# Two batches of retention one after the other, the first group's operands made within the second batch, and a new order of conversions, norm and banks

## The reference, cut to what matters

```python
# retention: q, k, v are (2 batches, 8 heads, 768 tokens, 64)
for t in range(S):
    state = gamma * state + einsum('bhd,bhe->bhde', k[:, :, t], v[:, :, t])
    y[:, :, t] = scale * einsum('bhd,bhde->bhe', q[:, :, t], state)
x = y.transpose(0, 2, 1, 3).reshape(1536, 512)
# first feed-forward layer, 512 -> 2048 -> 512
h = x @ w_in
x = (h * sigmoid(1.702 * h)) @ w_out
# norm and second, gated layer, 512 -> 1536 -> 512
xn = x / sqrt(mean(x * x) + 1e-6) * rms_g
g = xn @ w_gate
out = (g * sigmoid(g) * (xn @ w_val)) @ w_out2
```

## Time and profile before

| | us |
|---|---|
| median of three executions | 650.26 (646.29 to 654.38) |
| the profiled execution | 644.55 |
| its span | 642.8 |
| TensorE (PE) busy | 596.5, 93% |
| TensorE's weight loads (PEld) busy | 562.3, 87% |
| VectorE (DVE) busy | 348.4, 54% |
| ScalarE (ACT) busy | 309.9, 48% |
| GpSimd (POOL) busy | 172.4, 27% |

### The profile page before, as it was taken

The page is one execution under the profiler, slowest core; times in us unless marked ns, Lnnn a source line. Parts: engine busy times, 40 slices in busy tenths (PEclk is TensorE's granted clock), DMA queues, the critical chain, the costliest instruction groups (busy, mean ns, idle before and its releaser), DMA issues.

```text
span 642.8 us, 9071 instructions
## 1 busy us (share of the span) xinstructions
PE 596.5 (93%) x3486; PEld 562.3 (87%) x3486; DVE 348.4 (54%) x477; ACT 309.9 (48%) x533; POOL 172.4 (27%) x187
## 2 busy tenths in 40 slices
PE   8996899899998887899998897799999999999997
PEld 7885899899998886799998896798888999998886
DVE  4557455447634544547644555666575466566331
ACT  2444566654425663544435553457343555555331
POOL 2643255100122443000122343352012355440000
PEclk9998799999999998999999898999999999999999
DMA  8881122322221121221312121223221522223102
GB/s 321 273 318 60 34 67 65 99 67 66 65 63 37 33 67 40 67 91 38 93 34 56 44 66 33 66 67 91 75 66 34 165 65 68 85 80 81 50 0 99
DMA packets 24219, 52.83 MB, mean 82 GB/s; under 512 B 1776, under 2 KB 1904, under 8 KB 24176
## 3 DMA queue, kind: packets, MB, share of 16 engines
q1 hardware_dynamic: 24176, 52.25, 26.5%
HBM read 49.09 MB, written 3.15 MB: 81 GB/s over the span
## 4 chain that ended last, share of the span: by engine, by line
PE 80%; DVE 7%; issue 4%; ACT 4%; POOL 3%; DMA 1%; SPq 1%; ACTq 0%; DVEq 0%; POOLq 0%
PE bank L432 36%; PE bank L383 13%; PE bank L386 12%; PE bank L385 12%; ACT w_hi L501 2%; PE bank L329 2%; PE bank L357 2%; DVE w_lo L657 2%; PE bank L338 2%; DVE x L745 1%; POOL raw L898 1%; PE bank L351 1%; DMA arena<-attn_in 1%; POOL raw L896 1%; PE bank L479 1%
## 5 line engine op out<-in xcount | busy, mean ns | idle before, releaser
L657 DVE TENSOR_TENSOR w_lo<-raw,w_hi 128x512 fp32r<-128x512 f32 (+2 forms) x148 | 141.1, 955 | 145.4 <-ACT w_hi L501 144.7
L383 PE MATMUL bank<-x_hi,w_hi 128*128 128x384 f32 x560 | 193.9, 346 | 27.0 <-DVE bank L707 18.5
L385 PE MATMUL bank<-x_lo,w_hi 128*128 128x384 f32 x560 | 189.5, 338 | 0.0
L386 PE MATMUL bank<-x_hi,w_lo 128*128 128x384 f32 x560 | 189.4, 338 | 0.0
L501 ACT ACTIVATE w_hi<-raw 128x512 fp32r<-128x512 f32 (+2 forms) x148 | 112.9, 766 | 59.0 <-POOL raw L898 35.0
L383 PEld LDWEIGHTS bank<-x_hi,w_hi 128*128 128x128 f32 x560 | 106.9, 191 | 35.0 <-DVE bank L707 25.0
L385 PEld LDWEIGHTS bank<-x_lo,w_hi 128*128 128x128 f32 x560 | 107.1, 191 | 0.7 <-issue 0.6
L386 PEld LDWEIGHTS bank<-x_hi,w_lo 128*128 128x128 f32 x560 | 106.9, 191 | 0.0
L530 ACT ACTIVATE g_hi<-arena 128x768 fp32r<-128x768 f32 x56 | 46.8, 844 | 105.5 <-PE bank L432 105.5
L692 DVE TENSOR_TENSOR g_lo<-arena,g_hi 128x768 fp32r<-128x768 f32 x56 | 53.2, 956 | 79.3 <-ACT g_hi L530 79.1
L896 POOL TENSOR_TENSOR raw<-raw 128x256 f32<-128x256 f32 x40 | 30.0, 750 | 240.4 <-DVE w_lo L657 240.4
(11 more groups left out here) (64 smaller groups left out, 613.7 us busy)
## 6 DMA issues: line engine op xcount, KB each, us to landing
raw<-w SPq DMA_DIRECT2D x68, 512.0 KB, 3.7
arena<-attn_in SPq DMA_DIRECT2D x24, 512.0 KB, 6.2
out<-x SPq DMA_DIRECT2D x1, 1536.0 KB, 6.4
out<-x SPq DMA_DIRECT2D x6, 256.0 KB, 2.0
arena<-tables SPq DMA_DIRECT2D x1, 518.0 KB, 5.4
arena<-tables SPq DMA_DIRECT2D x1, 256.0 KB, 7.4
ident<-ident_in SPq DMA_DIRECT2D x1, 64.0 KB, 9.9
gain<-gain_in SPq DMA_DIRECT2D x1, 2.0 KB, 10.4
```

What stands on the lines that cost most here:

```text
L383: pe.matmul(dst, w_hi[q][:, w], x_hi[:, x], start=start and kk == 0, stop=False, skip_group_check=True)
L385: pe.matmul(dst, w_hi[q][:, w], x_lo[:, x], start=False, stop=False, skip_group_check=True)
L386: mm = pe.matmul(dst, w_lo[q][:, w], x_hi[:, x], start=False, stop=kk == 1, skip_group_check=True)
L657: dve.tensor_tensor(w_lo[q % 3][:, dst], src, w_hi[q % 3][:, dst].bitcast(F32), ALU.subtract)\
```

## The change

1. Retention goes batch by batch: step a is chunk a % 6 of batch a // 6. State, k and q decays are counted anew; the increment k^T v is made for each head by itself, 8 matmuls of 64 x 64 in place of 4 of 128 x 128. Each batch's first chunk has no cross part, each batch's last no increment.
2. The seven operands of group 0 are made between the steps of the second batch, and the weights of unit 0 are split and lowered behind them.
3. Hidden units: on VectorE `c22` comes ahead of the lowering of the unit's weight pieces 1 and 2, which moves into the unit that uses them; TensorE waits for piece 2 only ahead of product 7. GpSimd makes its four sums without waiting for a lowering, two of them into columns of their own, and the raw buffers are two of 1792 columns.
4. The norm's steps stand two units later and are spread out; the diagonals are two VectorE instructions of 768 columns with a high and a low part, and the broadcast uses four fp32r matmuls. The second half of `normalise` moves into the first project unit.
5. The hidden tiles 0 and 1 are converted earlier in a pass's last hidden unit. `FIRST` takes banks 0, 1, 6, 2 ahead of product 4.

```diff
...
-FIRST = {1: (6, 7, 0, 1, 2, 4, 3, 5), 2: (6, 7, 0, 1, 2, 4)}
+FIRST = {1: (0, 1, 6, 2, 4, 3, 5, 7), 2: (0, 1, 6, 2, 4, 7)}
...
                     for p in range(PAIRS):
-                        mm = pe.matmul(val[par][:, cols(p, P)], k_dec[par][:, cols(p, P)], v[:, cols(p, P)],
-                                       start=True, stop=True)
+                        for h in range(2):
+                            mm = pe.matmul(val[m % 2][64 * h:64 * h + 64, cols(p, 64)],
+                                           k_dec[m % 2][:, cols(2 * p + h, 64)], v[:, cols(2 * p + h, 64)],
+                                           start=True, stop=True, skip_group_check=True)
...
-                pe.wait_ge(w_lo_done, lo_at[r] + 3)
+                pe.wait_ge(w_lo_done, lo_at[r] + 2)
                 pe.wait_ge(m1_copied, n + 1)
                 product(6, n, 2, 1, 2, T2, False)
                 product(2, n, 0, 0, 2, B21, False)
                 pe.wait_ge(m5_copied, n + 1)
                 product(3, n, 1, 1, 3, B22, False)
                 pe.wait_ge(u2_copied, n + 1)
+                pe.wait_ge(w_lo_done, lo_at[r] + 3)
                 product(7, n, 2, 1, 0, T3, False)
...
-                    mm = pe.matmul(bank[6 + th][:, 0:HALF], ones[:, :], diag[:, cols(th, HALF)], start=True, stop=True)
+                    pe.matmul(bank[6 + th][:, 0:HALF], ones_r[:, :], diag_hi[:, cols(th, HALF)],
+                              start=True, stop=False)
+                    mm = pe.matmul(bank[6 + th][:, 0:HALF], ones_r[:, :], diag_lo[:, cols(th, HALF)],
+                                   start=False, stop=True)
                 mm.then_inc(bcast_done, 1)
-                    if p in (1, 2) and j == 2:
+                    if p in (1, 2) and j == 4:
                         norm_totals(p - 1)
-                    if p in (1, 2) and j == 4:
+                    if p in (1, 2) and j == 6:
                         norm_bcast(p - 1)
...
+                for c in {3: (B11,), 4: (B21,), 7: (T1,), 8: (T2, B22), 9: (T3,), 10: (T4,)}.get(a, ()):
+                    split_x(0, c)
+                if a == 10:
                     split_w(0, 0)
-                    split_w(0, 1)
-                if s == 10:
-                    split_w(0, 2)
-            for c in (T1, T2, B22, T3, T4):
-                split_x(0, c)
+            split_w(0, 1)
+            split_w(0, 2)
...
+                    if last:
+                        split_g(p, 0)
...
+                    if last:
+                        split_g(p, 1)
...
-                    if p in (1, 2) and j < 2:
-                        squares(p - 1, j)
-                    if j == HIDDEN[layer] - 1:
-                        split_g(p, 0)
-                        split_g(p, 1)
+                    if p in (1, 2) and j < 4:
+                        squares(p - 1, j // 2, j % 2)
...
-                for t in range(SEQ // P):
-                    ins = dve.tensor_scalar(diag[:, cols(t, P)], ident[:, :], inv_rms[:, t:t + 1], None, ALU.mult)
...
+                for diag, inv in ((diag_hi, inv_hi[:, :].bitcast(F32)), (diag_lo, inv_lo[:, :])):
+                    ins = dve.tensor_tensor(diag[:, :].rearrange("p (t q) -> p t q", q=P),
+                                            ident[:, :].unsqueeze(1).to_broadcast(shape),
+                                            inv.unsqueeze(2).to_broadcast(shape), ALU.mult)
                 ins.then_inc(diag_done, 1)
...
+                if c > 0:
+                    dve.wait_ge(state_decayed, (CHUNKS - 2) * g + c)
...
+                if a == 4:
                     lower_x(0, B11)
+                elif a == 5:
                     lower_x(0, B21)
-                if s == 10:
+                elif a == 6:
+                    sum_x(0, T1)
+                elif a == 7:
+                    sum_x(0, T2)
+                    lower_x(0, T1)
+                elif a == 8:
+                    lower_x(0, T2)
+                    lower_x(0, B22)
+                elif a == 9:
+                    lower_x(0, T3)
+                    sum_x(0, T4)
+                elif a == 10:
+                    lower_x(0, T4)
                     lower_w(0, 0)
-                    lower_w(0, 1)
-            lower_w(0, 2)
-            sum_x(0, T1)
-            lower_x(0, T1)
-            sum_x(0, T2)
-            lower_x(0, T2)
-            lower_x(0, B22)
-            lower_x(0, T3)
-            sum_x(0, T4)
-            lower_x(0, T4)
 
...
                         c22(n - 1)
-                        if is_val(n - 1):
-                            gate_tile(n - 1, 2)
-                            gate_tile(n - 1, 3)
-                    lower_next(r, 0)
+                    lower_w(r, 1)
+                    if j > 0 and is_val(n - 1):
+                        gate_tile(n - 1, 2)
+                    lower_w(r, 2)
+                    if j > 0 and is_val(n - 1):
+                        gate_tile(n - 1, 3)
+                    if p in (1, 2):
+                        if j in (2, 4):
+                            add_squares(p - 1, j // 2 - 1)
+                        if j == 5:
+                            means(p - 1)
+                        if j == 6:
+                            diagonals(p - 1)
+                        if j == 7:
+                            normalise(p - 1, 0)
+                    if j == HIDDEN[layer] - 1:
+                        lower_g(p, 0)
+                    lower_next(r)
                     if is_val(n):
                         gate_tile(n, 0)
-                    lower_next(r, 1)
                     c12(n)
                     if is_val(n):
                         gate_tile(n, 1)
-                    lower_next(r, 2)
-                    if p in (1, 2):
-                        if j < 2:
-                            add_squares(p - 1, j)
-                        if j == 3:
-                            means(p - 1)
-                        if j == 4:
-                            diagonals(p - 1)
-                        if j in (5, 6):
-                            normalise(p - 1, j - 5)
                     if j == HIDDEN[layer] - 1:
-                        lower_g(p, 0)
                         lower_g(p, 1)
...
-                    lower_next(r, 0)
-                    for f in (2 * j + 2, 2 * j + 3):
-                        if f < TILES[layer]:
-                            lower_g(p, f)
-                        if f == 2 and is_val(n):
-                            gate_tile(n, 3)
+                        if p in (1, 2):
+                            normalise(p - 1, 1)
+                    lower_next(r)
+                    if j < PROJECT[layer] - 1:
+                        lower_g(p, 2 * j + 2)
...
                 pool.tensor_tensor(s1, a21, a22, ALU.add).then_inc(w_sums, 1)
                 pool.wait_ge(w_sums, sums_at[r] + 1)
+                pool.tensor_tensor(s2, s1, a11, ALU.subtract).then_inc(w_sums, 1)
+                pool.wait_ge(w_sums, sums_at[r] + 2)
+                pool.tensor_tensor(s4, a12, s2, ALU.subtract).then_inc(w_sums, 1)
+
                 pool.tensor_tensor(a21, a11, a21, ALU.subtract).then_inc(w_sums, 1)
-
-                pool.wait_ge(w_lo_done, lo_at[r] + 1)
-                pool.wait_ge(w_sums, sums_at[r] + 2)
-                pool.tensor_tensor(a11, s1, a11, ALU.subtract).then_inc(w_sums, 1)
-                pool.wait_ge(w_sums, sums_at[r] + 3)
-                pool.tensor_tensor(a12, a12, a11, ALU.subtract).then_inc(w_sums, 1)
```

More of the change, by code:

```diff
@@ L68, in transformer_kernel @@
         w_lo = [sb(f"w_lo{i}", 1024, F32R) for i in range(3)]
-        raw = [sb(f"raw{i}", 1280) for i in range(3)]
+        raw = [sb(f"raw{i}", 1792) for i in range(2)]
         t3 = sb("t3", OPERAND)
@@ L294, in _ @@
             sp.dma_start(gain[:, :], gain_in).then_inc(const_in, 16)
-            for s in range(SLOTS, STEPS):
-                sp.wait_ge(y_done, s - SLOTS + 1)
-                load(s)
-                load_kv(s)
-                if s >= STEPS - 3:
-                    load_weights(s - STEPS + 3)
-            for r in range(3, len(units)):
+            for a in range(SLOTS, STEPS):
+                sp.wait_ge(y_done, a - SLOTS + 1)
+                load(a)
+                load_kv(a)
+                if a in (7, 9):
+                    load_weights((a - 7) // 2)
+            for r in range(2, len(units)):
                 load_weights(r)
@@ L571, in squares @@
                     act.wait_ge(sum_sq_done, 2 * i + th)
-                for dh in range(2):
-                    act.activation(square[dh][:, :], x32[i][:, cols(2 * dh + th, OPERAND)], ACT.Square)\
-                       .then_inc(squared, 1)
+                act.activation(square[dh][:, :], x32[i][:, cols(2 * dh + th, OPERAND)], ACT.Square)\
+                   .then_inc(squared, 1)
             act.wait_ge(ones_set, 1)
@@ L607, in _ @@
                     n, r = h_at[p, j], at["hidden", p, j]
+                    last = j == HIDDEN[layer] - 1
```

(30 more changed lines are left out.)

222 lines of the change are left out of this document (125 added, 97 removed).

## The result

The changed kernel takes 600.28 us (median of four, 596.87 to 600.82) against 649.19 us (646.29 to 654.38) for the kernel before. The ratio is 0.923, 95% interval 0.917 to 0.929: 7.7% faster. The forecast was 608.5 us in a range of 598 to 624.

The account below looks back on a forecast made before the run. TensorE bounds the kernel: its work plus 46.3 us standing still. Terms A to E, 3.9 + 18.0 + 11.7 + 5.6 + 2.2 = 41.4 us off 644.55, give 603.2 profiled; with ratio 1.0089, 608.5 us; range 598 to 624.

Parts of the forecast that it names:

- A: Attention and first products: product 6 starts 3.1 us earlier, half clock costs 2.5 less, a new stretch 1.7 more: -3.9 us.
- B: Hidden units: with `c22` first on VectorE, TensorE's ten waits for it (18.5 us) go, 0.5 left: -18.0 us.
- The chain: Attention from step 3's output on: VectorE and ScalarE work with hand-overs sets the pace, 35.1 us, ending at 61.3 us.
- rival 3: Better than the sum: clock does not fall, increments cost 0.50, surplus of runs over profile halves: 602.5 us; chance 0.14.
- rival 1: Attention's end is dearer: operand instructions 1.48 us instead of 0.94 beside GpSimd, longer half clock: 616 us; chance 0.18.
- the +0.54 I took from one row: Attention: a VectorE operand instruction took 1.48 us instead of 0.94 while GpSimd worked.
- C: Norm: diagonals' waits go (-7.3 us) and the broadcast of 2.90 us shrinks to 0.7, twice: -11.7 us.
- D: Starts of project phases: waits of 3.1 + 3.0 us go, 0.5 left: -5.6 us.
- E: Clock: the half-clock stretch at 355.4 goes (-1.7), and the ends of two others beside the broadcast: -2.2 us.
- Two raw buffers: Weight loads: two raw buffers for three, costed at nothing, with slack of 3.9 us.
- Rival 4: Two raw buffers set the pace: landings of 10 us throughout cost 48 us over 40 hidden units: 656 us; chance 0.03.

Follow-up runs that it names:

- e6: Changed kernel with GpSimd's decays of k and q cut to one head from step 7 on: profiled 596.35 us in one run.
- e2: Changed kernel with weight pieces 1 and 2 lowered ahead of `c22` again: profiled 597.98 us, median 599.64.
- e7: Changed kernel with the norm's VectorE steps ahead of `c22` again, in their new units: profiled 616.24 us, median 615.43.
- e8: e2 with GpSimd's sums in place as before, so that they wait for a lowering: profiled 606.19 us, median 605.94.
- e11: e8 with the norm as before too, in its old units, keeping split diagonals and short broadcast: 640.4 us in one run.
- e4: Changed kernel with the norm's broadcast as float32 matmuls of six single diagonals, in the new place: span 596.9 us, one run.
- e3: Changed kernel with hidden tiles 0 and 1 split and lowered late, at the end of the last hidden unit: span 601.2 us, one run.
- e5: Changed kernel with T1, T2, B22 lowered one step after their split and T3, T4 lowered behind attention: profiled 590.0 us, median 590.60.
- e10: e5 with weight piece 1 of unit 0 split and lowered ahead of T3: profiled 587.24 us, median 588.81.

## Why the prediction was right

Every wait and every stretch at half clock that the prediction named behind attention went away, and the sum was 6.3 us too high for the profiled execution (603.2 against 596.9). Two terms were mis-sized, in opposite directions: A gained 1.4 us less than forecast and B 7.0 more, so that the sum came this close is in a small part luck. And B's cause is only in part the one it gave.

**A, attention** (forecast -3.9). Measured -2.5: product 6 did not come 3.1 us earlier but at the same time, and the half clock behind it went. The chain was forecast to end at 61.3 us and ended at 64.7, and the wait ahead of the last output was not one of over 4 us but two of 3.74 and 2.63. The increment took 0.61 us, between the forecast's 0.85 and the 0.50 of rival 3. The chain's form was right: state, decay, split, lowering in one step, with the clock falling at the end. Too small were the prices under GpSimd (0.94 for instructions of 1.80 and 2.07 and, on average, 1.73), which was rival 1's point, and the half clock: 10.3 us with attention's own matmuls in it, not 3.4. The Trainium skill's rule in "SBUF — State Buffer", "Who interferes with whom", that the two engines shut each other out for a whole instruction, fits the 2.07 better than the +0.54 I took from one row. e6 shows that the price alone was worth 1.3 us.

**B, `c22`** (forecast -18.0). The waits went whole, as forecast. The size was wrong: I read 18.5 us from the matmuls' list, and the loads' list has 25.0. This is the mis-sized term, and nearly all of the sum's error. The cause given, squares, pieces or `normalise` in front of `c22`, is only a part: with the pieces there (e2) the loads wait 1.1 us at `c22`, with the norm's steps there (e7) 1.8. It took the pieces with GpSimd's old sums to bring back 9.8 us (e8), and these with the norm in its old units to bring back 23.6 (e11). The sums that no longer wait for a lowering, which the prediction costed at nothing, are thus half of a cure.

**C, norm** (-11.7): 7.3 us of waits went, the broadcast is 0.7 us for 2.90, as priced; e7 shows the diagonals' wait (4.8 us of it, in the new units) and e4 the broadcast's price.

**D, project starts** (-5.6): all 6.1 us went; e3 brings them back.

**E, clock** (-2.2): no half clock behind 64.6 us until the end, as forecast. That the clock stays up after a wait of 2.89 us, as the prediction read from one row, does not hold in general: e11 has a wait of the same 2.89 us and 6.6 us at half clock, from its last 0.8 us on. **Two raw buffers** cost nothing: TensorE has no wait for a transfer in pass 0 to 3. Rival 4 had nothing.

The last step, from the profiled time to the median with the ratio 1.0089, was too large; it was 1.0057 here.

## What to carry to other kernels

Look for a bottleneck engine's stalls in both of its lists, matmuls and weight loads: many stalls under the length of a record's overlap show only in the second. On an in-order engine, put what the bottleneck waits for first and periodic side work behind it; here the place of a few norm steps was worth 15 us by the medians (19 by the profiles) and the rewrite of attention 2 at most. An edit that one experiment shows to be worth nothing may still be one of two cures of the same stall: undo such edits together as well. When work is moved between the steps of a recurrence, give it a step of distance between the engines (split in one, lower in the next), or it lengthens the recurrence instead of filling its gaps; and move no more of it there than the gaps hold (e5 did both at once).

## What the runs showed of the hardware

A VectorE sum of two operands in SBUF took 2.07 us beside GpSimd's full instructions and 0.96 beside their narrow ones (e6).

TensorE's clock fell at the end of a wait of 3.74 us and stayed at 1.2 GHz for 10.3 us, in which TensorE was busy for 7.4 and waited once more, 2.63 us. The length of a wait does not tell by itself whether the clock falls. After 2.89 us it stayed up in the kernel before and was at half for 6.6 us in e11; e11 also has 3.4 us at half, from 259.0, behind a wait of 1.93 us at 257.65. In e10 no wait was above 1.5 us and the granted clock was 1.00 for the whole span, but e5, whose waits are as short, had this stretch early in attention, behind waits of 1.23, 0.38 and 1.30 us:

```profile
13.50:16.70 3.20, 3.20 (x33) 2.87 (x31) 0.06 (x1) 1.24 (x4) 2.24 (x3) 0.53 0.92 333
```

The repeated run of the changed kernel had a span of 598.5 at a mean clock of 0.982 against 595.1 at 0.991: its stretch at attention's end lasted 13.7 us for 10.3, and it had another of 6.7 us from 10.9. Part of the spread between the runs goes with such stretches, not all of it: a third run had 0.991 and a span of 597.5.
